# Eight heads' scores from two row blocks of TensorE, and three chunks' decays by load, in an mLSTM and MLP-mixer kernel

## The reference

```
for t in range(S):
    m_new = maximum(f[t] + m, i[t])
    C = exp(f[t] + m - m_new) * C + exp(i[t] - m_new) * outer(v[t], k[t])
    n = exp(f[t] + m - m_new) * n + exp(i[t] - m_new) * k[t]
    y[t] = sigmoid(o[t]) * (C @ q[t]) / maximum(abs(n @ q[t]), 1)
x = y as [B, S, 320]
u = x + (relu(x^T @ w_tok1) @ w_tok2)^T        # 768 -> 256 -> 768
out = u + relu(u @ w_ch1) @ w_ch2              # 320 -> 1536 -> 320
```

## Time and profile before

| what | value |
|---|---|
| median of 3 runs | 455.25 us |
| profiled execution, its span | 455.49 us, 453.8 us |
| TensorE busy | 439.6 us (97% of the span) |
| VectorE, ScalarE, GpSimd busy | 255.6, 209.1, 208.3 us |
| scores products (line 1077), passes | 144, two to each of 72 products |
| chain that ended last | TensorE 85%, VectorE 5%, issue 4%, ScalarE 4% |
| bytes moved | 47.38 MB, mean 104 GB/s |

### The profile page before, as it was taken

How to read it: one execution, slowest core, us unless ns; L and a number is a source line. 1 busy time by engine, 2 the same in 40 slices (tenths; PEclk the granted TensorE clock), 3 DMA queues, 4 the chain that set the end, 5 groups by cost and what they waited for, 6 DMA issues and landing times.

```text
span 453.8 us, 9518 instructions
## 1 busy us (share of the span) xinstructions
PE 439.6 (97%) x3463; PEld 407.6 (90%) x3463; DVE 255.6 (56%) x592; ACT 209.1 (46%) x517; POOL 208.3 (46%) x293
## 2 busy tenths in 40 slices
PE   8899999999999999899999999999999999999996
PEld 3588988999999989799999998899999998999996
DVE  7689865777765356776674237666665326213122
ACT  3666459666554247654552137655652213211120
POOL 7535421789886333888861204798883000000000
PEclk9899999999999999999999999999999999999999
DMA  7557990443344415434454013534310010000101
GB/s 211 195 168 217 348 263 27 119 129 111 103 131 146 127 43 166 143 92 131 124 154 143 1 44 102 150 120 142 126 61 1 1 43 2 0 1 0 46 1 43
DMA packets 36616, 47.38 MB, mean 104 GB/s; under 512 B 3356, under 2 KB 29082, under 8 KB 36570
## 3 DMA queue, kind: packets, MB, share of 16 engines
q1 hardware_dynamic: 35674, 45.76, 33.4%
q10 hardware_dynamic: 896, 1.02, 0.6%
HBM read 42.73 MB, written 4.03 MB: 103 GB/s over the span
## 4 chain that ended last, share of the span: by engine, by line
PE 85%; DVE 5%; issue 4%; ACT 4%; DMA 1%; DVEq 0%; POOL 0%; POOLq 0%; ACTq 0%
PE pC L1165 32%; PE pA L1236 7%; PE pA L1237 7%; PE pA L1238 7%; PE pS L1077 6%; PE pA L1165 5%; PE pY L1134 4%; PE pA L1240 3%; PE pA L1241 3%; PE pC L1015 2%; PE pY L1113 2%; PE pN L1089 2%; DVE gb L856 1%; PE pA L1195 1%; DMA x<-o_gate_dram 1%
## 5 line engine op out<-in xcount | busy, mean ns | idle before, releaser
L988 DVE SCALAR_TENSOR_TENSOR h_lo<-pA,h_hi 128x384 fp32r<-128x384 f32 x96 | 53.5, 557 | 147.9 <-ACT h_hi L760 147.9
L760 ACT ACTIVATE h_hi<-pA 128x384 fp32r<-128x384 f32 x96 | 46.8, 488 | 138.7 <-PE pA L1241 138.6
L1165 PE MATMUL pC<-wc_hi,h_hi 128*128 128x320 f32 x288 | 94.1, 327 | 1.1 <-DVE wc_lo L846 1.0
L1165 PE MATMUL pC<-wc_lo,h_hi 128*128 128x320 f32 x288 | 88.7, 308 | 0.0
L1165 PE MATMUL pC<-wc_hi,h_lo 128*128 128x320 f32 x288 | 88.4, 307 | 0.0
L494 POOL TENSOR_TENSOR gb<-gb,pb 128x384 f32<-128x384 f32 (+1 forms) x54 | 49.1, 909 | 63.9 <-ACT pb L628 63.4
L1236 PE MATMUL pA<-uT_hi,wc_hi 128*128 128x384 f32 x192 | 65.2, 340 | 0.3 <-DVE wc_lo L846 0.3
L1237 PE MATMUL pA<-uT_lo,wc_hi 128*128 128x384 f32 x192 | 64.7, 337 | 0.0
L1238 PE MATMUL pA<-uT_hi,wc_lo 128*128 128x384 f32 x192 | 64.3, 335 | 0.0
L1165 PEld LDWEIGHTS pC<-wc_hi,h_hi 128*128 128x128 f32 x288 | 54.0, 188 | 2.3 <-DVE h_lo L988 1.3
L1165 PEld LDWEIGHTS pC<-wc_lo,h_hi 128*128 128x128 f32 x288 | 54.2, 188 | 0.1
(11 more groups left out here) (135 smaller groups left out, 881.6 us busy)
## 6 DMA issues: line engine op xcount, KB each, us to landing
gb<-g_dram SPq DMA_DIRECT2D x18, 512.0 KB, 3.9
kv<-kvN_dram SPq DMA_DIRECT2D x24, 324.0 KB, 4.0
kd<-kT_dram SPq DMA_DIRECT2D x24, 180.0 KB
qz<-qT_dram SPq DMA_DIRECT2D x72, 60.0 KB
out_dram<-u SPq DMA_DIRECT2D x24, 160.0 KB, 1.9
qd<-qT_dram SPq DMA_DIRECT2D x20, 180.0 KB, 2.6
gq<-g_dram SPq DMA_DIRECT2D x45, 60.0 KB
wc_raw<-w_ch_dram SPq DMA_DIRECT2D x6, 384.0 KB, 6.1
```

Of the source, the lines that this page charges most:

```text
L760: nc.scalar.activation(h2[0][:, slot % 2], pA[slot % 2][:, 0:HALF], ACT.Relu).then_inc(h2_hi, 1)
L988: nc.vector.scalar_tensor_tensor(h2[1][:, slot % 2], pA[slot % 2][:, 0:HALF], 0.0, h2[0][:, slot % 2].bitcast(F32), ALU.max, ALU.subtract) ...
L1165: ins = mm(dst, a[p], b[q], start=first and n == 0, stop=last and n == 2)
```

## The change

Keys and queries are stored in one tensor `kq`, even heads on rows 0 to 39, odd heads on rows 64 to 103 (from a new input of the host's layout). A chunk's scores are made at its first step, all eight heads, with eight fp32 products of 128 columns, alternately on the lower and the upper block of rows; even heads go to `pS`, odd ones to `pC[0]` in the first batch and to `pN` in the others. The zeros in `qz` and their setting are gone. They wait until VectorE has read all three groups of the chunk before, and in batches 1 to 3 until the states' products are read from `pN`. VectorE reads each group with two instructions, one for each bank. In batches 1 to 3 the states' products of groups 0, 1 and 2 move: group 0 at the chunk's second step, groups 1 and 2 at its third. In the first batch the decays of chunks 3 to 5 come by broadcast load and GpSimd's mask, as in the others; TensorE's spreading of them is left out. The loads' order on SyncE changes, and the second chunk's loads wait for the output gate's.

```diff
-        kd = sb("kd", [ROWS, R, NG, L])
-        qz = sb("qz", [ROWS, R, NG, GH, L])
+        kq = sb("kq", [128, R, 2, H // 2, L])
...
-        def scores_bank(ba, m):
-            return [pS, pC[0]][m % 2] if ba == 0 else pS
+        def scores_place(ba, head):
+            pair, odd = divmod(head, 2)
+            return (pC[0] if ba == 0 else pN) if odd else pS, pair * L
+        def state_place(ba, g):
+            col = L if ba > 0 and g == NG - 1 else 0
+            return pN[0:HEADS[g] * D, col:col + HEADS[g] * E1]
+        def scores_of(ba, head):
+            where, col = scores_place(ba, head)
+            return where[:, col:col + L]
...
+        def states_in(ba, m):
+            if ba == 0:
+                return [m - 1] if 1 <= m <= STEPS - NG else []
+            c, g = divmod(m, NG)
+            if c >= NC - 1 or g == 0:
+                return []
+            return [m - 1] if g == 1 else [m - 1, m]
...
                 if n >= R:
-                    sp.wait_ge(s_mm, NG * (n - R + 1))
+                    sp.wait_ge(s_mm, n - R + 1)
                 ready = qk_in[r]
-                queries = qT[ba, c]
-                sp.dma_start(kd[:, r], kT[ba, c]).then_inc(ready, 16)
-                for j in range(GH):
-                    rows_j = slice(j * D, (j + 1) * D)
-                    sp.dma_start(qz[rows_j, r, :, j, :], queries[rows_j, :, :]).then_inc(ready, 16)
+                for odd in range(2):
+                    sp.dma_start(kq[64 * odd:64 * odd + D, r], kq_pairs[ba, c, odd]).then_inc(ready, 16)
...
+            load_scores(0, 0)
             load_values(0, 0)
-            sp.wait_ge(mem_ready, 1)
-            load_scores(0, 0)
+            for half in range(2):
+                sp.wait_ge(o_in[half], 16)
             load_chunk(0, 1)
             for n in range(4):
                 load_weight(n)
-            load_chunk(0, 2)
-            load_weight(4)
-            load_chunk(0, 3)
-            load_weight(5)
+            load_scores(0, 2)
             sp.wait_ge(g_ready, len(SEGMENTS))
             g_rows = G_row.rearrange("p (c t) -> p c t", t=L)
             sp.dma_start(g_dram[:, 0:NH, :].rearrange("c p t -> p c t"), g_rows).then_inc(g_out, 16)
             sp.dma_start(g_dram[:, NH:NH + 1, :].rearrange("c p t -> p c t"), g_rows[0:1]).then_inc(g_pad_out, 16)
-            load_chunk(0, 4)
+            load_scores(0, 3)
+            load_rest(0, 2)
+            load_weight(4)
+            sp.wait_ge(g_out, 16)
+            sp.wait_ge(g_pad_out, 16)
+            load_decays(0, 3)
+            load_scores(0, 4)
+            load_decays(0, 4)
+            load_rest(0, 3)
+            load_weight(5)
+            load_scores(0, 5)
+            load_decays(0, 5)
+            load_rest(0, 4)
             load_weight(6)
-            load_chunk(0, 5)
+            load_rest(0, 5)
...
+                    if FIRST_LOADED <= c + 1 < NC:
+                        mask(0, c + 1)
...
-                    if c >= Q:
-                        act.wait_ge(y_mm, NG * (c - Q + 1))
-                act.wait_ge(g_mm, m + 1)
+                if c < FIRST_LOADED:
+                    act.wait_ge(g_mm, m + 1)
+                else:
+                    act.wait_ge(first_masked, m - NG * FIRST_LOADED + 1)
                 for j in range(HEADS[g]):
                     head = GH * g + j
-                    last = nc.scalar.activation(gb[:, c % Q, head, :], pA[m % 2][:, j * L:(j + 1) * L], ACT.Exp,
+                    tile = gb[:, c % Q, head, :]
+                    sums = pA[m % 2][:, j * L:(j + 1) * L] if c < FIRST_LOADED else tile
+                    last = nc.scalar.activation(tile, sums, ACT.Exp,
...
-                tile = gb[:, c % Q, GH * g:GH * g + n, :]
-                dve.wait_ge(s_mm, k + 1)
+                dve.wait_ge(s_mm, NC * ba + c + 1)
+                if ba > 0 and c < NC - 1 and g > 0:
+                    dve.wait_ge(n_mm, NG * (NC - 1) * ba + NG * c + (1 if g == 1 else NG))
                 dve.wait_ge(e_exp, k + 1)
-                nc.vector.tensor_tensor(tile, scores_bank(ba, m)[:, 0:n * L].rearrange("p (h t) -> p h t", h=n), tile,
-                                        ALU.mult).then_inc(p_ready, 1)
+                for odd in range(2):
+                    heads = [h for h in range(GH * g, GH * g + n) if h % 2 == odd]
+                    tile = gb[:, c % Q, heads[0]:heads[-1] + 1:2, :]
+                    where, col = scores_place(ba, heads[0])
+                    sums = where[:, col:col + len(heads) * L].rearrange("p (h t) -> p h t", t=L)
+                    last = nc.vector.tensor_tensor(tile, sums, tile, ALU.mult)
+                last.then_inc(p_ready, 1)
...
+            def chunk_scores(ba, c):
+                n = NC * ba + c
+                r = c % R
+                pe.wait_ge(qk_in[r], 16 * QK_DMAS * (ba * (NC // R) + c // R + 1))
+                if n > 0:
+                    pe.wait_ge(p_ready, NG * n)
+                if ba > 0:
+                    pe.wait_ge(n_read, states(ba, c - 1))
+                for head in range(H):
+                    pair, odd = divmod(head, 2)
+                    rows = slice(64 * odd, 64 * odd + D)
+                    last = mm(scores_of(ba, head), kq[rows, r, 0, pair, :], kq[rows, r, 1, pair, :],
+                              start=True, stop=True)
+                last.then_inc(s_mm, 1)
...
-                if ks != 0:
+                if ba == 0 and ks != 0:
                     pe.wait_ge(n_read, ks)
-                mm(pN[0:n * D, 0:n * E1], kv[:, r, GH * g * D:(GH * g + n) * D],
+                if ba > 0:
+                    pe.wait_ge(p_ready, STEPS * ba + NG * c + (1 if g == 0 else 2))
+                    if g > 0:
+                        pe.wait_ge(n_read, NG * (NC - 1) * ba + NG * c + 1)
+                mm(state_place(ba, g), kv[:, r, GH * g * D:(GH * g + n) * D],
...
-                if m < STEPS:
-                    step_scores(ba, m)
+                if m < STEPS and m % NG == 0:
+                    chunk_scores(ba, m // NG)
                 if ba == 0:
                     if m in (1, 4):
                         gate_transposes((1, 4).index(m) + 1)
                     for k in (2,) if m == 0 else (3, 4) if m == 1 else (m + LEAD,):
                         if k < STEPS:
-                            spread_decays(k)
+                            if k < NG * FIRST_LOADED:
+                                spread_decays(k)
                             if k == 2:
                                 keep_warm(WARM_THIRD)
                             if k % NG == 2 and k // NG + 1 < NC:
                                 spread_query_decays(k // NG + 1)
-                if 1 <= m <= STEPS - NG:
-                    step_state(ba, m - 1)
+                for done in states_in(ba, m):
+                    step_state(ba, done)
...
```

More of the change, by code:

```diff
@@ L79, in step_in, with program @@
     return slot - BEHIND if b == 0 else slot + AHEAD
-def program(nc, qT, kT, kvN, i_gate, f_gate, o_gate, w_tok1, w_tok2, w_ch1, w_ch2, out):
+def program(nc, kq_pairs, qT, kvN, i_gate, f_gate, o_gate, w_tok1, w_tok2, w_ch1, w_ch2, out):
     ctx = ExitStack()
@@ L928, in attention @@
                     scores(ba, m)
-                if 1 <= m <= STEPS - NG:
-                    state(ba, m - 1)
+                for done in states_in(ba, m):
+                    state(ba, done)
                 c = chunk_at(ba, m, 0) if (ba, m) != (0, NG - 1 + FIRST_LAG) else None
@@ L1289 @@
     arrays = {
-        "qT": rows(q), "kT": rows(k),
+        "kq_pairs": np.ascontiguousarray(np.stack([paired(k), paired(q)], axis=4)),
+        "qT": rows(q),
         "kvN": np.ascontiguousarray(np.concatenate([tokens(k).reshape(B, S, DM), values.reshape(B, S, H * E1)], axis=2)),
```

31 lines of the change are left out of this document (10 added, 21 removed).

## The result

The kernel became **slower: 465.0 us** (median of 4 runs, 463.74 to 465.62) against 454.9 us; ratio 1.021, 95% interval 1.017 to 1.026. Forecast was 449.0 us. The profiled execution took 464.5 us and has a span of 462.6 us. Ratios and intervals, but not the medians, leave out slow executions: two of e6_fill_spread (462.8 and 471.8 us) and one of the kernel before (856 us, in the session of e13 and e14).

What follows compares the result with a forecast made beforehand. It took TensorE's own stream to bound batches 1 to 3, and TensorE and VectorE, both full, the first batch. 455.5 - 10.1 (scores) + 1.8 (VectorE's waits) + 1.8 (first batch) = 449.0 us, range 441 to 462.

Steps and rivals of the forecast that it cites:

- Scores in batches 1 to 3: TensorE's scores there: passes on the two row blocks overlap, 1.73 to 1.17 us a chunk, -10.1 us over 18 chunks.
- rivals on weight loads: Scores products: weight loads do not overlap, each pass waits for its own; 461.9 us, slower; chance 0.20.
- a dear change of rows: TensorE around the scores: switching rows costs 0.3 us each way despite overlap; 456.2 us, no change; chance 0.15.
- VectorE's waits in batches 1 to 3: TensorE waits longer for VectorE, whose score reads grow 0.30 us a chunk: 0.1 us a chunk, +1.8 us.
- Start, -1.0: First batch's start: second chunk's keys and queries no longer compete with the output gate's load, -1.0 us.
- `kv` behind the decays, +3.0 for two chunks: First batch, SyncE: `kv` loads queue behind the next chunk's decays, 1.5 us for each of chunks 3 and 4, +3.0.
- masks hidden: First batch, GpSimd: 1.7 us of decay masks a chunk stay hidden while the loads come in time, no cost.
- against it: ScalarE is a step or two ahead: First batch: the argument against late loads holding it up, that ScalarE runs a step or two ahead; no size.
- Reads +1.5: First batch: VectorE, already full, takes 0.30 us more for score reads in each of five chunks, +1.5 us.
- TensorE lighter -1.0: First batch: TensorE loses score work and decay spreading; -0.5 us in each of chunks 1 and 2, -1.0.
- The clock: First batch, 31 to 43 us: granted clock must stay at 1.00; at half the batch loses more, no size given.
- The rival on late loads: First batch: its loads hold it up, three chunks each lose 1.5 us more, +4.5; 453.5 us, no change; chance 0.12.

Runs made afterwards that it cites:

- e6_fill_spread: Changed kernel, first batch's decays all spread by TensorE, first keys and queries held behind GpSimd's set-up, two filling products a step from step 6: 457.1 us.
- e13: e8 with heads dealt to the row blocks by groups, so VectorE reads a chunk's scores in four instructions instead of six: 449.3 us.
- e14: Kernel before, with only the states' products and VectorE's reads of them moved to the chunk's second and third steps in batches 1 to 3: 454.4 us.
- e9: e8 with the odd heads' multiplication on VectorE left out in batches 1 to 3, so the computation is incomplete: 448.3 us.
- e3: Changed kernel with the first loads in the order of before and no wait for the output gate: 467.4 us.
- e5: Changed kernel with the load of chunk 0's keys and queries held until GpSimd's set-up is done, behind the output gate's load: 465.4 us.
- e7: Kernel before, with the first batch's decays of chunks 3 to 5 loaded and masked as in the change, scores as before: 470.6 us.
- e10: e7 with four unused bf16 products of 512 columns added on TensorE per first-batch step from the eighth on: 464.5 us.
- e1: Changed kernel with four unused bf16 products of 512 columns added on TensorE per first-batch step from step 7 on: 460.7 us.
- e2: Changed kernel with the decays of chunks 3 to 5 of the first batch spread by TensorE again, without their loads and masks: 466.9 us.
- e11: Changed kernel with e1's filling, `kv` loads issued ahead of the next chunk's decays, and e5's held first load together: 457.1 us.
- e8: Kernel before in the whole first batch, with the change's row-block scores in batches 1 to 3 alone: 451.6 us.

## Why the prediction was wrong

**Right.** Scores in batches 1 to 3: overlap of the blocks, 0.2 us for the change of rows or less, 1.19 us a chunk for 1.17. The rivals on weight loads and on a dear change of rows are refuted: the loads of two 40-row operands run beside each other, sixteen in 1.09 us. The Trainium skill (TensorE: Matmul & The Clock Gate, "Part 3: Packing small matmuls") says that a load overlaps with products in flight only where the row groups differ; the trace agrees on the overlap of the two blocks, and the "only" no run here tests. Counted from start to start by line, the scores fell from 30.3 to 19.7 us in the three stages, and the change of rows stands behind the last `hidden` product with 18 x 0.1 = 1.8 us: -8.9 us, forecast -10.1. Set against the profiled execution of before, the whole miss of some 15.5 us is then this 1.2, 3.4 in VectorE's waits, 10.4 in the first batch and 0.3 in the tail.

**Mis-sized: VectorE's waits in batches 1 to 3.** Forecast +1.8 us. Since the stages gained 3.7 us of 8.9, 5.2 us went back. By the same count the states' part of the values grew by 2.8 us, the states' products by 1.8, what follows the last `hidden` by 1.0 beyond the change of rows. The timeline of the changed kernel shows the first of them:

```profile
106.83 1.25 DVE L904 TENSOR_TENSOR pb<-gb,pb 128x384 bf16<-128x384 f32 x1
```

```profile
108.15 0.62 PE L1181 MATMUL pY<-vb,pb 128*128 128x41 bf16 x18 [0.52 <-DVE pb L904]
```

This row shows the wait and not its cause: the same multiplication takes 1.26 us at this place in the kernel before as well, and 0.56 in e9. Of the 5.2, e9 (2.2 us, with more work away than the change had added) and e14 (1.1 to 2.1 us) account for some 3.3 to 4.3; the rest is open, and so is 1 us of the 5.2 itself.

The forecast's shape was wrong too, an equal 0.1 us in every chunk. Three slots in a row (a chunk) from the first `hidden` product of the slot take:

| slots of the stage | before | after | e9_half_reads |
|---|---|---|---|
| batch 1's stage, 4 to 6 | 11.28 | 11.56 | 11.23 |
| 7 to 9 | 12.22 | 12.41 | 11.75 |
| 10 to 12 | 12.84 | 13.30 | 12.64 |
| 13 to 15 | 12.56 | 12.17 | 12.20 |
| batch 3's stage, 7 to 9 | 12.59 | 12.18 | 12.18 |
| 10 to 12 | 12.55 | 12.14 | 12.14 |

Where the stage runs evenly, 0.4 us of the scores' 0.5 arrives in each chunk, and leaving out half of VectorE's reads changes nothing: it is not waited for. The loss stands in a stage's first slots, above all in batch 1's. The forecast priced the added 0.30 us of reads and held the moved states' products for free; e14's stages say that they are not, though its median stays at that of before.

**Failed: the first batch, +12.2 us for +1.8.** The step that failed is the forecast's belief that the decays' masks are hidden and that the loads cost 1.5 us a chunk, together with a sum that has no term for engines taking turns and none for the clock. By term:

- *Start, -1.0*: it was +1.5. The change takes away VectorE's zeros that held the first keys' and queries' load back, and puts that load ahead; it then competes with the output gate's. e3 (12.78 us, with chunk 1's loads beside it too) and e5 (8.07 us) show it both ways. I counted what no longer competes, not what newly does.
- *`kv` behind the decays, +3.0 for two chunks; masks hidden "while the loads come in time"*: they did not. Chunk 3's decays stood 5.7 us from issue to mask, and chunk 3's state product came 8.0 us after the release where I had set 6.5 as the bound. The forecast's "against it: ScalarE is a step or two ahead" failed: ScalarE was ahead because the spread sums were three steps ahead in a bank, and the change takes just that away. e7 and e10: 9.5 to 10.8 us by itself at nearly full clock, filling included.
- *Reads +1.5, TensorE lighter -1.0*: these price amounts of work. What cost beyond them was that eight scores at once make TensorE and VectorE take turns: in e6 at most 3.3 us, of which 1.9 us can be read as such waits.
- *The clock*: named among the things to watch, but in no sum and no rival. The forecast itself let TensorE wait there. It fell to half for 30.7 us and cost 3.5 us or more (e1). What holding it brings depends on what else waits: up to the first `hidden` 6.8 us from e7 to e10, and 9.8 from e2 to e6, there with e5's start in it.

Undone one after another, in the order e1, e11, e6, the parts are 3.5 us clock, 2.1 order of the loads, 3.4 decays by load (58.09 to 54.71), 3.3 eight at once. That they sum to the 12.2 us shows nothing, since each is the step from one kernel of a chain to the next; in another order the shares differ, and from e11 to e6 the filling also falls from 52 products (13.9 us) to 18. What the runs do show is that either part alone makes a hole into which the clock falls (e7 the loads; e2 the scores with the new start), that e7's +14.7 us at the first MLP product exceeds the whole change's +10.4, and that with the first batch as before nothing is lost (e8). Why the loads alone cost more than together with the rest is not shown; SyncE's order is another there, with chunk 4's keys and queries behind chunk 3's `kv`. How the 12.2 us split stays open. The rival on late loads had the right place and half of the first batch's price (+4.5 beside the +1.8).

## What to carry to other kernels

Splitting a short contraction over two row blocks with separate banks makes the products as cheap as the arithmetic says, even with an fp32 weight load per pass; but of 8.9 us saved only 2.7 to 3.7 reached the time here. It belongs where TensorE alone is full. Dealing the blocks so that the reader needs fewer instructions (e13) is worth trying, though its 0.3 us in the stages is not clear of noise. In a stage where several engines are full, do not ask which of them gets lighter, but who was ahead of whom and by what buffer: a value made three steps ahead and one loaded behind a buffer's release are not the same thing at equal work. Whoever makes TensorE wait for microseconds must put the lower clock into the sum as a case of its own.

## What the runs showed of the hardware

- Two 40-row fp32 products of 128 columns on rows 0 to 39 and 64 to 103 run side by side with their weight loads: a pair of passes each 0.11 us, sixteen passes and the way back 1.09 us. At the lower clock the pairs stand 0.21 us apart (44.13, 44.34 us in the changed kernel).
- The change between blocks and whole columns costs about 0.1 us where it could be read.
- The granted clock stayed at 1.2 GHz for 30.7 us, in which TensorE was busy 99%, after one hole of some 6 us (3.88 us busy), and in e10 for 3.4 us only after a hole of like size (3.07 of 6 us busy). In all six kernels with a stretch of 30 us or more it rose only after the first MLP product (65.9 for 61.76 us here, 68.6 for 63.69 in e5); of the falls after 20 us, only e10's ended inside the attention, with filling products of 512 bf16 columns between. What decides is open.
- Chunk 3's `kv` load (324 KB) landed after 6.4 us where a 512 KB broadcast load had been issued 0.45 us ahead of it, and after 3.3 us in the kernel before, without one. The medians over the whole span (512 KB: 5.3 us for 3.9; `kv`: 4.8 for 4.0) do not come from the first batch alone: e8, whose first batch is that of before, has 5.3 us as well.
